# Attention and two MLPs on one core: the value product's halves go through DRAM and are added by GpSimd

## The chip, the cores and the metric

The kernel runs on one core of a Trainium2 chip. The metric is the device time of one execution in microseconds; smaller is better. The kernel before takes 773.73 us (median of 3 runs, 772.16 to 774.55).

## The reference

Three stages follow each other: causal attention over 4 batches x 8 heads with 576 positions and 64 columns a head, an MLP with a softmax gate and a layer norm (512 to 1024 to 512), and an MLP that takes the larger of three products (512 to 768 to 512).

```python
scores = scale * q @ k.T                      # 32 heads, S = 576, D = 64
bias = -(cum[:, :, :, None] - cum[:, :, None, :])
scores = where(causal, -1e9, scores + minimum(bias, 0.0))
attn = softmax(scores);  x = attn @ v         # then to (2304 tokens, 512)
h = x @ w_in                                  # (2304, 1024)
solu = h * softmax(h)
x = (solu - mean) / sqrt(var + 1e-6) * g_ln @ w_out
out = maximum(maximum(x @ w1, x @ w2), x @ w3) @ w_out2
```

## The kernel before

All products run with float32 data that are split in a high part, which is exact in the matmul's format, and a low part; one product takes two or three matmuls. The order of each engine is written out by hand, with semaphores between the engines.

The attention runs in slots, one per head. In slot t TensorE computes the scores of head t (and the first part of those of head t+1, `scores_4`), transposes the probabilities of head t-1 in four groups (`turn` 0 to 3, banks 3 and 4 of PSUM) and multiplies those of head t-2 with the values (`values`, lines 436 to 442). The values lie in `v_hl` with their high part in columns 0 to 63 and their low part in 64 to 127, so that the product has the high half in partitions 0 to 63 and the low half in 64 to 127 of a bank. Columns 0 to 319 of a head go to bank 6 (`PV_A`), 320 to 575 to bank 7 (`PV_B`).

The two halves are joined so: ACT copies the low half of each bank to SBUF (`copy_vlo_a`, `copy_vlo_b`, lines 800 to 812, at the end of its slot), and VectorE adds it to the high half in PSUM and writes the sum into `xT` (`add_a`, `add_b`, lines 1030 to 1042, one slot later, between its row maxima and its `pt_low`). `xT` holds x transposed: head 2j+r of a batch lies in partitions 64r to 64r+63 of block j. TensorE waits for these adds before it writes the banks again (lines 482 and 491).

Per slot VectorE further does `q_low`, five row maxima (`row_max`) and four `pt_low`; ACT does four `pt_high`, the split of v, and five exps; GpSimd does `qk_high` and `k_low` of head t+1 and `split_v` of head t-1 (lines 695 to 702). In the last 8 pairs of slots of its loop it also splits a piece of w_in (`split_win`).

SP issues all transfers, in one queue, in the order of its program. `reload(t, par)` (lines 314 to 325) waits until GpSimd and VectorE are done with head t-2, issues the load of q and k of head t in two copies of 288 KB (one for each half of the partitions), waits for `v_lo_ready` (GpSimd's `split_v` of head t-3), issues the two v loads of head t-1, waits for the scores of head t-2 and issues the small aux load. After each pair of reloads a block of the first MLP's weights is loaded (512 KB of w_in four times, 256 KB of w_out eight times). At the end (lines 359 to 377) the reloads of heads 28 to 31 are written out, with the row sums stored to DRAM and loaded back broadcast (`store_rinv`, `load_rinv`) between them. In slot 28 (RTURN) TensorE turns the row sums and VectorE inverts them.

The first MLP works on 6 groups of 384 tokens. GpSimd multiplies a group with the inverse row sums (`divide`, lines 718 to 723; the first one ahead of the last v split of the attention), ACT and VectorE split it (`x_high`, `x_low`), TensorE multiplies (`hidden`), and GpSimd normalizes (`normalize`) before TensorE transposes again. ACT's first `x_high` stands ahead of its slot 32.

Of the kernel before, what the change touches and what calls it, by code (L numbers as in the profile page):

```python
# [5 lines left out]
F32 = mybir.dt.float32  # L6
# [30 lines left out]
def attention_and_mlp(nc, qkT, v, s, w_in, w_out, g_ln, w1, w2, w3, w_out2, out):  # L37
# [25 lines left out]
    QA = 3 * P - PAD  # L63
    QB = S - QA

    PV_A = [(0, J0 + PAD, J0 + 3 * P, 0), (1, J1, J1 + 2 * P, PAD), (2, J2, J2 + P, PAD + P)]
    PV_B = [(0, J0 + 3 * P, J0 + 5 * P, 0), (1, J1 + 2 * P, J1 + 4 * P, 0), (2, J2 + P, J2 + 3 * P, 0),
            (3, J3, J3 + 2 * P, 0), (4, J4, J4 + P, P)]
# [12 lines left out]
    aux_dram = nc.dram_tensor("aux_dram", (HEADS, 8, S), F32, kind="Internal").ap()  # L81
    rsum_dram = nc.dram_tensor("rsum_dram", (HEADS, S), F32, kind="Internal").ap()

    with ExitStack() as ctx:
# [29 lines left out]
        xg = sb(ab_, "xg", [P, KC, GT])  # L114
        win_lo = sb(ab_, "win_lo", [P, KC, FF], F32R)


        with ExitStack() as a:
# [6 lines left out]
            vlo_a = sb(a, "vlo_a", [D, QA])  # L125
            vlo_b = sb(a, "vlo_b", [D, QB])

# [80 lines left out]
        vloa_copied = sem("vloa_copied")  # L208
        vlob_copied = sem("vlob_copied")
        xa_done = sem("xa_done")  # L210
        xb_done = sem("xb_done")
# [72 lines left out]
        def _(sp):  # L284
# [29 lines left out]
            def reload(t, par, known=None):  # L314
# [10 lines left out]
                load_aux(t, par)  # L325

            reload(2, 0, 2)
            reload(3, 1)

            def reload_pair(pair):  # L330
                reload(2 * pair, 0)
                reload(2 * pair + 1, 1)


            with sp.Fori(2, 2 + KC) as pair:
                reload_pair(pair)
                sp.dma_start(stage[:, bass.ds(pair * FF - 2 * FF, FF)], w_in[bass.ds(pair * P - 2 * P, P), :]).then_inc(w_loaded, 16)
# [69 lines left out]
        def _(pe):  # L407
# [51 lines left out]
            def slot(t, par, known):  # L459
# [17 lines left out]
                if live(known, 2):  # L477
                    pe.wait_ge(v_hi_ready, t - 1)
                    pe.wait_ge(v_lo_ready, t - 1)
                    pe.wait_ge(pt_lo_done, 4 * (t - 1))  # L480
                    if known != 2:
                        pe.wait_ge(xa_done, t - 2)
                    values(t, par, 6, PV_A)
# [5 lines left out]
                if live(known, 2):  # L489
                    if known != 2:  # L490
                        pe.wait_ge(xb_done, t - 2)
# [82 lines left out]
            pe.wait_ge(xa_done, HEADS)  # L574
            pe.wait_ge(xb_done, HEADS)
# [70 lines left out]
        def _(pool):  # L646
# [90 lines left out]
            pool.wait_ge(xa_done, HB)  # L737
            pool.wait_ge(xb_done, HB)
# [4 lines left out]
            pool.wait_ge(xa_done, 2 * HB)  # L743
            pool.wait_ge(xb_done, 2 * HB)
# [8 lines left out]
            pool.wait_ge(xa_done, HEADS)  # L753
            pool.wait_ge(xb_done, HEADS)
# [18 lines left out]
        def _(act):  # L773
# [33 lines left out]
            def copy_vlo_b(t, par, known):  # L807

                if known != 2:
                    act.wait_ge(xb_done, t - 2)  # L810
                act.wait_ge(pv_done, 2 * (t - 2) + 2)
                act.activation(vlo_b[:, :], ps[D:P, 7, 0:QB], ACT.Copy).then_inc(vlob_copied, 1)

            def slot(t, par, known):
# [160 lines left out]
        def _(dve):  # L975
# [49 lines left out]
            def columns(t, par, known):  # L1025

                pair = (t - 4 + par) // 2 if known is not None else (t - 4 + par) >> 1
                return (pair % KC) * TOKENS + (pair // KC) * S

            def add_a(t, par, known):  # L1030

                flat = xT[:, :, :].rearrange("p c t -> p (c t)")
                dve.wait_ge(vloa_copied, t - 2)
                dve.tensor_tensor(flat[D * (1 - par):D * (2 - par), bass.ds(columns(t, par, known), QA)], ps[0:D, 6, 0:QA],  # L1034
                                  vlo_a[:, :], ALU.add).then_inc(xa_done, 1)

            def add_b(t, par, known):

                flat = xT[:, :, :].rearrange("p c t -> p (c t)")
                dve.wait_ge(vlob_copied, t - 2)  # L1040
                dve.tensor_tensor(flat[D * (1 - par):D * (2 - par), bass.ds(columns(t, par, known) + QA, QB)], ps[0:D, 7, 0:QB],
                                  vlo_b[:, :], ALU.add).then_inc(xb_done, 1)

# [10 lines left out]
            def slot(t, par, known):  # L1054
# [6 lines left out]
                if live(known, 3):  # L1061
# [186 lines left out]
```

## Time and profile before

| | |
|---|---|
| median of 3 runs | 773.73 us |
| profiled execution | 776.48 us |
| its span, first to last instruction | 774.2 us |
| mean granted TensorE clock | 0.989 of full speed |
| TensorE / its weight loads busy | 720.6 / 664.9 us (93% / 86%) |
| VectorE busy | 418.0 us (54%) |
| ACT busy | 328.5 us (42%) |
| GpSimd busy | 226.3 us (29%) |
| DMA | 45.26 MB, mean 58 GB/s |

The busy shares are averages over the whole span. In the 40 equal slices of the page VectorE is at 9 tenths from the third to the eleventh slice (attention) and between 1 and 6 tenths after the thirteenth (the MLPs), and GpSimd is at 4 to 9 tenths in the first eleven. TensorE is at 8 to 9 in both stages. The DMA engines are at 4 to 6 tenths in the attention, at 0 to 2 later.

### The profile page before, as it was taken

The page shows a single profiled execution, that of the slowest core. Times are in us where ns is not written, and L with a number is a line of the kernel's source. Part 1 is how long each engine was busy: PE and PEld are TensorE (multiplying, and loading weights), DVE is VectorE, ACT ScalarE, POOL GpSimd, SP SyncE. Part 2 cuts the span into 40 slices and gives each one's busy share as a digit, 9 for nine tenths or more (in the row PEclk, how much of TensorE's full clock was granted, in tenths as well). Part 3 has the DMA queues.
Part 4 walks back from the last instruction along what each step waited for, and adds up shares of the span by engine and source line. Part 5 has one row for each costly group of instructions (what it writes and reads, how often), then busy time and mean ns, then how long its engine had stood idle before and what let it go on. Part 6 is the DMA issues. An engine that isn't in the chain of part 4 may idle for free.

```text
span 774.2 us, 12663 instructions
## 1 busy us (share of the span) xinstructions
PE 720.6 (93%) x4248; PEld 664.9 (86%) x4248; DVE 418.0 (54%) x766; ACT 328.5 (42%) x795; POOL 226.3 (29%) x242
## 2 busy tenths in 40 slices
PE   2798898999889899999999999999999999999997
PEld 1787787888777788889898989999989999899995
DVE  8799999999995684635354463612313213132120
ACT  1688788888874443414232242412112112121111
POOL 6665768989742641304040200000000000000000
PEclk9799999999999999999999999999999999999999
DMA  6555455555341101105200022000010010000101
GB/s 136 118 140 153 130 144 131 141 133 137 95 91 42 42 13 29 42 1 145 60 0 0 0 81 83 1 14 28 1 41 1 1 40 1 30 11 0 41 0 41
DMA packets 46579, 45.26 MB, mean 58 GB/s; under 512 B 22164, under 2 KB 37652, under 8 KB 46516
## 3 DMA queue, kind: packets, MB, share of 16 engines
q1 hardware_dynamic: 46548, 44.86, 21.9%
q8 instruction: 18, 0.29, 0.2%
q14 instruction: 13, 0.11, 0.1%
HBM read 39.43 MB, written 5.38 MB: 58 GB/s over the span
## 4 chain that ended last, share of the span: by engine, by line
PE 65%; DVE 10%; DMA 7%; issue 6%; POOL 5%; SPq 4%; ACT 2%; DVEq 0%; POOLq 0%; ACTq 0%
PE ps L606 10%; PE ps L605 10%; PE ps L604 10%; DMA qk_raw<-in_qk_dram 7%; PE ps L536 4%; PE ps L538 4%; PE ps L537 4%; PE ps L524 3%; PE ps L526 3%; PE ps L525 3%; PE ps L617 3%; PE ps L619 3%; PE ps L618 3%; DVE nmax L1007 2%; POOL qk_b L676 2%
## 5 line engine op out<-in xcount | busy, mean ns | idle before, releaser
L606 PE MATMUL ps<-x_lo,w_hi 128*128 (+1 forms) x432 | 144.4, 334 | 0.0
L604 PE MATMUL ps<-x_hi,w_hi 128*128 128x384 f32 x432 | 144.3, 334 | 0.0
L605 PE MATMUL ps<-x_hi,w_lo 128*128 128x384 f32 x432 | 144.3, 334 | 0.0
L788 ACT ACTIVATE probs<-ps,nmax 128x576 f32<-128x576 f32 (+4 forms) x160 | 82.6, 530 | 17.2 <-DVE nmax L1007 17.2
L798 ACT ACTIVATE pt_hi<-ps 128x512 fp32r<-128x512 f32 (+1 forms) x128 | 69.8, 569 | 34.5 <-PE ps L433 28.3
L433 PE MATMUL ps<-ident,probs 128*128 128x128 f32 x480 | 74.3, 286 | 10.4 <-DVE pt_lo L1014 5.8
L440 PE MATMUL ps<-pt_hi,v_hl 128*128 128x256 f32 (+2 forms) x256 | 67.7, 294 | 16.5 <-DVE xT L1034 13.6
L604 PEld LDWEIGHTS ps<-x_hi,w_hi 128*128 128x128 f32 x432 | 81.1, 188 | 0.2
L605 PEld LDWEIGHTS ps<-x_hi,w_lo 128*128 128x128 f32 x432 | 81.1, 188 | 0.2
L606 PEld LDWEIGHTS ps<-x_lo,w_hi 128*128 128x128 f32 x432 | 81.1, 188 | 0.0
L1014 DVE TENSOR_TENSOR pt_lo<-ps,pt_hi 128x512 fp32r<-128x512 f32 (+1 forms) x128 | 78.0, 649 | 4.8 <-ACT pt_hi L798 3.9
L415 PE MATMUL ps<-k_a,q_a 128*128 128x288 f32 (+2 forms) x192 | 64.3, 342 | 14.5 <-DVE rinvT L1052 14.1
L1007 DVE TENSOR_REDUCE nmax<-ps 128x1 f32<-128x576 f32 (+4 forms) x160 | 72.7, 484 | 4.6 <-PE ps L420 3.2
L933 ACT ACTIVATE m_hi<-stage 128x384 fp32r<-128x384 f32 x36 | 18.9, 525 | 124.9 <-DVE stage L1193 124.9
L440 PEld LDWEIGHTS ps<-pt_hi,v_hl 128*128 128x128 f32 x256 | 49.3, 193 | 21.9 <-issue 14.3
L536 PE MATMUL ps<-lnT_hi,wout_hi 128*128 128x384 f32 x192 | 64.4, 335 | 2.7 <-DVE lnT_lo L1138 2.7
L433 PEld LDWEIGHTS ps<-ident,probs 128*128 128x128 f32 x480 | 53.3, 145 | 15.8 <-issue 6.9
L1195 DVE TENSOR_TENSOR m_lo<-stage,m_hi 128x384 fp32r<-128x384 f32 x36 | 20.1, 558 | 82.2 <-ACT m_hi L933 82.2
L538 PE MATMUL ps<-lnT_lo,wout_hi 128*128 128x384 f32 x192 | 64.2, 335 | 0.0
L537 PE MATMUL ps<-lnT_hi,wout_lo 128*128 128x384 f32 x192 | 64.2, 334 | 0.0
L441 PE MATMUL ps<-pt_lo,v_hl 128*128 128x256 f32 (+2 forms) x256 | 61.0, 286 | 0.0
L524 PE MATMUL ps<-win_hi,x_hi 128*128 128x512 f32 x144 | 57.5, 399 | 2.8 <-DVE ln L1122 2.1
(102 smaller groups left out, 1441.5 us busy)
## 6 DMA issues: line engine op xcount, KB each, us to landing
qk_raw<-in_qk_dram SPq DMA_DIRECT2D x64, 288.0 KB, 4.2
rinvB<-rsum_dram SPq DMA_DIRECT2D x24, 192.0 KB, 3.8
stage<-in_moe_w_dram SPq DMA_DIRECT2D x18, 256.0 KB, 4.4
out_dram<-stage SPq DMA_DIRECT2D x18, 256.0 KB, 2.0
v_raw<-in_v_dram SPq DMA_DIRECT2D x32, 128.0 KB, 2.4
stage<-in_moe_w_out_dram SPq DMA_DIRECT2D x14, 256.0 KB, 2.7
stage<-in_moe_w_in_dram SPq DMA_DIRECT2D x4, 512.0 KB, 3.6
aux_dram<-setup SPq DMA_DIRECT2D x1, 576.0 KB, 4.5
```

The lines of the kernel that those rows point to most:

```text
L433: mm = pe.transpose(ps[:, GBANK[g], P * n:P * (n + 1)], probs[1 - par][:, o:o + P], ident[:, :])
L440: pe.matmul(dst, v_hl[par][:, j, :], pt_hi[par][:, a0:a1], start=(n == 0), stop=False)
L524: pe.matmul(dst, x_hi[ab][:, c, :], win_hi[:, c, cols], start=(c == 0), stop=False)
L536: pe.matmul(dst, wout_hi[:, f, cols], lnT_hi[:, f, :], start=(f == 0), stop=False)
L537: pe.matmul(dst, wout_lo[:, f, cols], lnT_hi[:, f, :], start=False, stop=False)
L538: mm = pe.matmul(dst, wout_hi[:, f, cols], lnT_lo[:, f, :], start=False, stop=(f == FB - 1))
L604: pe.matmul(dst, w_hi[f][:, i, c, :], x2_hi[par][:, c, :], start=(c == 0), stop=False)
L605: pe.matmul(dst, w_lo[f][:, i, c, :], x2_hi[par][:, c, :], start=False, stop=False)
L606: mm = pe.matmul(dst, w_hi[f][:, i, c, :], x2_lo[:, c, bass.ds(g * GT, GT)], start=False, stop=(c == KC - 1))
L788: act.activation(dst, SCORES[c], ACT.Exp, bias=nmax[par][:, c:c + 1], accum_out=sums_all[:, c, bass.ds(t, 1)]).then_inc(exp_done, 1)
L1007: dve.tensor_reduce(nmax[par][:, c:c + 1], SCORES[c], AX_XY if c == NCH - 1 else AX_X, ALU.max, negate=True).then_inc(max_done, 1)
L1014: dve.tensor_tensor(pt_lo[1 - par][:, o:o + n], ps[:, GBANK[g], 0:n], f32(pt_hi[1 - par][:, o:o + n]), ALU.subtract).then_inc(pt_lo_done, 1)
```

## The change

Each product is no longer joined on its way out of PSUM. The banks are divided at column 288 instead of 320. ACT copies all 128 partitions of a bank, both halves together, into a new SBUF tile `halves` (two of them, by parity): the first bank's copy stands ahead of three of the slot's exps, the second's at the end of the slot. Before the first of these ACT waits for the store of the head two before. SP stores each head's tile to a new DRAM tensor `x_dram` (288 KB) in `reload`, behind the aux load, five heads later, and reads it back near the end of the attention: the high halves straight into `xT`, one batch at a time (`load_xa`, two transfers of 576 KB), and the low halves group by group into a new tile `xb` (`load_xb`, four transfers of 192 KB). GpSimd adds `xb` to `xT` before each `divide`. VectorE's two adds per head are gone. TensorE waits for ACT's copies instead of VectorE's adds before it writes a bank again. The scratch for dynamic DMAs is set to 4096.

```diff
+    PV_A = [(0, J0 + PAD, J0 + PAD + HALF, 0), (1, J1, J1 + HALF - PAD, PAD), (2, J2, J2 + HALF - P - PAD, P + PAD)]
...
                 sp.wait_ge(scores_done, 3 * (t - 1))
                 load_aux(t, par)
+                if known is None or known >= 5:
+                    store_x(t - 5, 1 - par)
+
+            def store_x(h, par):
+
+                sp.wait_ge(xa_copied, h + 1)
+                sp.wait_ge(x_copied, h + 1)
+                rows = x_dram[bass.ds(h, 1)].rearrange("a p s -> (a p) s")
+                sp.dma_start(rows, halves[par][:, :, :].rearrange("p a b -> p (a b)")).then_inc(x_stored[par], 16)
+
+            def load_xa(b):
+
+                for par in range(2):
+                    sp.wait_ge(x_stored[par], 16 * (b + 1) * HB // 2)
+                for par in range(2):
+                    src = x_dram[HB * b:HB * (b + 1), 0:D, :].rearrange("(j r) d s -> r d j s", r=2)[par]
+                    sp.dma_start(xT[D * par:D * (par + 1), :, S * b:S * (b + 1)], src).then_inc(xa_loaded, 16)
+
+            def load_xb(g):
+
+                if g > 0:
+                    sp.wait_ge(x_added, g)
+                for part in range(2):
+                    b_, s0 = divmod(g * GT + part * GT // 2, S)
+                    for par in range(2):
+                        src = x_dram[HB * b_:HB * (b_ + 1), D:P, s0:s0 + GT // 2].rearrange("(j r) d t -> r d j t", r=2)[par]
+                        dst = xb[D * par:D * (par + 1), :, part * GT // 2:(part + 1) * GT // 2]
+                        sp.dma_start(dst, src).then_inc(xb_loaded, 16)
...
             reload(HEADS - 4, 0)
+            load_xa(0)
             reload(HEADS - 3, 1)
+            load_xb(0)
             reload(HEADS - 2, 0)
+            load_xa(1)
             sp.wait_ge(rinv_done, 1)
             store_rinv(slice(0, LAST))
             reload(HEADS - 1, 1)
@@
             load_rinv(0)
             sp.wait_ge(v_lo_ready, HEADS - 2)
             load_v(HEADS - 1, 1)
+            store_x(HEADS - 5, 1)
+            load_xa(2)
+            store_x(HEADS - 4, 0)
+            store_x(HEADS - 3, 1)
             sp.wait_ge(xg_ready, 1)
             load_rinv(1)
+            load_xb(1)
+            store_x(HEADS - 2, 0)
+            store_x(HEADS - 1, 1)
+            load_xa(3)
...
             for g in range(2, NG):
                 sp.wait_ge(xg_ready, g)
                 load_rinv(g)
+                load_xb(g)
...
             def divide(g, known):
 
+                cols = xT[:, :, bass.ds(g * GT, GT)]
+                pool.wait_ge(xb_loaded, 64 * (g + 1))
+                pool.tensor_tensor(cols, cols, xb[:, :, :], ALU.add).then_inc(x_added, 1)
                 pool.wait_ge(rinvB_loaded, 64 * (g + 1))
                 if known != 0:
                     pool.wait_ge(x_lo_ready, 3 * g)
-                pool.tensor_tensor(xg[:, :, :], xT[:, :, bass.ds(g * GT, GT)], rinvB[:, :, :], ALU.mult).then_inc(xg_ready, 1)
+                pool.wait_ge(x_added, g + 1)
+                pool.tensor_tensor(xg[:, :, :], cols, rinvB[:, :, :], ALU.mult).then_inc(xg_ready, 1)
...
-            def copy_vlo_a(t, par, known):
-
-                if known != 2:
-                    act.wait_ge(xa_done, t - 2)
+            def copy_half_a(t, par, known):
+
+                if known is None or known >= 4:
+                    act.wait_ge(x_stored[par], (t - 2 - par) * 8)
                 act.wait_ge(pv_done, 2 * (t - 2) + 1)
-                act.activation(vlo_a[:, :], ps[D:P, 6, 0:QA], ACT.Copy).then_inc(vloa_copied, 1)
+                act.activation(halves[par][:, 0, :], ps[:, 6, 0:HALF], ACT.Copy).then_inc(xa_copied, 1)
...
                 if live(known, 1):
                     pt_high(2, t, par, known)
                     pt_high(3, t, par, known)
+                if live(known, 2):
+                    copy_half_a(t, par, known)
                 if live(known, 0):
                     exp(t, par, known, 0)
                     exp(t, par, known, 2)
                     exp(t, par, known, 1)
                 if live(known, 2):
-                    copy_vlo_a(t, par, known)
-                    copy_vlo_b(t, par, known)
+                    copy_half_b(t, par, known)
...
-                if live(known, 3):
-                    add_a(t, par, known)
...
-                if live(known, 3):
-                    add_b(t, par, known)
```

Before the first normalization GpSimd now waits for all four `load_xa`, where it waited for the last adds.

## Rows read from the trace of the kernel before

**Rows 1.** The page, part 1: busy us, share of the span, instructions
```profile
PE 720.6 (93%) x4248; PEld 664.9 (86%) x4248; DVE 418.0 (54%) x766; ACT 328.5 (42%) x795; POOL 226.3 (29%) x242
```

**Rows 2.** Windows, 140 to 180 us: busy us by engine, clock, DMA share
```profile
140.00:180.00 40.00, 37.36 (x286) 33.75 (x285) 39.09 (x75) 35.43 (x105) 35.58 (x38) 1.00 0.53 138
```

**Rows 3.** Waits, 100 to 200 us, of all engines and of SP: total, times, longest
```profile
POOL q_a L670 <- DMA qk_raw<-in_qk_dram: 10.3, 7, 2.8
...
PE ps L440 <- DVE xT L1034: 4.4, 10, 0.9
...
SPq L296 <- POOL v_hl L680: 41.7, 15, 4.5
```

**Rows 4.** Chain that ended last, 139 to 153 us: start, us, what
```profile
139.20 4.28 DMA qk_raw<-in_qk_dram
...
143.74 0.08 POOL q_a L670
...
147.52 0.87 POOL v_hl L680
...
148.55 0.47 SPq L296
...
149.90 0.27 SPq L301
...
150.50 0.36 SPq L340
...
151.56 0.50 SPq L292
...
152.26 4.21 DMA qk_raw<-in_qk_dram
```

**Rows 5.** Timeline of SP's queue, 78 to 100 us: start, us
```profile
81.67 0.47 SPq L296 DMA_DIRECT2D v_raw<-in_v_dram  x1
...
95.94 0.47 SPq L296 DMA_DIRECT2D v_raw<-in_v_dram  x1
```

**Rows 6.** Chain that ended last, 78 to 123 us
```profile
85.58 5.29 DMA qk_raw<-in_qk_dram
```

**Rows 7.** The page, part 6: DMA issues, KB each, median us to landing
```profile
out_dram<-stage SPq DMA_DIRECT2D x18, 256.0 KB, 2.0
...
stage<-in_moe_w_out_dram SPq DMA_DIRECT2D x14, 256.0 KB, 2.7
stage<-in_moe_w_in_dram SPq DMA_DIRECT2D x4, 512.0 KB, 3.6
```

**Rows 8.** Groups by form: count, busy us, mean ns, idle before
```profile
L723 POOL TENSOR_TENSOR xg<-xT,rinvB 128x1536 f32<-128x1536 f32 x6 | 21.0, 3507 | 82.5 <-DVE x_lo L1091 82.5
...
L805 ACT ACTIVATE vlo_a<-ps 64x320 f32<-64x320 f32 x32 | 13.9, 434 | 6.8 <-PE ps L441 6.1
...
L812 ACT ACTIVATE vlo_b<-ps 64x256 f32<-64x256 f32 x32 | 11.8, 369 | 1.2 <-PE ps L441 1.2
L1034 DVE TENSOR_TENSOR xT<-ps,vlo_a 64x320 f32 x24 | 11.6, 484 | 0.7
...
L1182 DVE TENSOR_TENSOR x_lo<-xT,x_hi 128x1536 fp32r<-128x1536 f32 x6 | 10.5, 1758 | 4.1 <-ACT x_hi L920 4.1
...
L1041 DVE TENSOR_TENSOR xT<-ps,vlo_b 64x256 f32 x24 | 9.9, 413 | 0.4
```

**Rows 9.** Timeline of ACT, 139 to 153 us: start, us, [idle before, releaser]
```profile
149.83 0.98 ACT L798 ACTIVATE pt_hi<-ps 128x512 fp32r<-128x512 f32 x2 [0.59 <-PE ps L433]
```

**Rows 10.** Timelines of SP, GpSimd and ACT at the end of the attention
```profile
196.42 1.11 SPq L292 DMA_DIRECT2D qk_raw<-in_qk_dram x2
...
202.88 0.67 POOL L670 TENSOR_SCALAR q_a<-qk_raw 128x576 fp32r<-128x576 f32 x1
...
231.41 3.49 POOL L723 TENSOR_TENSOR xg<-xT,rinvB 128x1536 f32<-128x1536 f32 x1
...
235.69 0.62 ACT L857 ACTIVATE x_hi<-xg 128x512 fp32r<-128x512 f32 x1
```

More of the change, by code:

```diff
@@ L81, in attention_and_mlp @@
     aux_dram = nc.dram_tensor("aux_dram", (HEADS, 8, S), F32, kind="Internal").ap()
+    x_dram = nc.dram_tensor("x_dram", (HEADS, P, S), F32, kind="Internal").ap()
     rsum_dram = nc.dram_tensor("rsum_dram", (HEADS, S), F32, kind="Internal").ap()
@@ L114, in attention_and_mlp @@
         xg = sb(ab_, "xg", [P, KC, GT])
+        xb = sb(ab_, "xb", [P, KC, GT])
         win_lo = sb(ab_, "win_lo", [P, KC, FF], F32R)
@@ L124, in attention_and_mlp @@
             nmax = [sb(a, f"nmax{i}", [P, NCH]) for i in range(2)]
-            vlo_a = sb(a, "vlo_a", [D, QA])
-            vlo_b = sb(a, "vlo_b", [D, QB])
+            halves = [sb(a, f"halves{i}", [P, 2, HALF]) for i in range(2)]
             q_a = [sb(a, f"q_a{i}", [P, SP], F32R) for i in range(2)]
@@ L207, in attention_and_mlp @@
         pv_done = sem("pv_done")
[L208 to L211, printed above, removed]
+        xa_copied = sem("xa_copied")
+        x_copied = sem("x_copied")
+        x_stored = [sem(f"x_stored{i}") for i in range(2)]
+        xa_loaded = sem("xa_loaded")
+        xb_loaded = sem("xb_loaded")
+        x_added = sem("x_added")
         sums_turned = sem("sums_turned")
@@ L325, in reload, with reload_pair, load_win @@
                 load_aux(t, par)
-            reload(2, 0, 2)
[L328 to L335, printed above, removed]
+                if known is None or known >= 5:
[20 more added lines that the diff above has]
+                        sp.dma_start(dst, src).then_inc(xb_loaded, 16)
+            reload(2, 0, 2)
+            reload(3, 1, 3)
+            def reload_pair(pair, known=None):
+                reload(2 * pair, 0, known)
+                reload(2 * pair + 1, 1, known and known + 1)
+            def load_win(pair):
+                sp.dma_start(stage[:, bass.ds(pair * FF - 2 * FF, FF)], w_in[bass.ds(pair * P - 2 * P, P), :]).then_inc(w_loaded, 16)
+            reload_pair(2, 4)
+            load_win(2)
+            with sp.Fori(3, 2 + KC) as pair:
                 reload_pair(pair)
-                sp.dma_start(stage[:, bass.ds(pair * FF - 2 * FF, FF)], w_in[bass.ds(pair * P - 2 * P, P), :]).then_inc(w_loaded, 16)
+                load_win(pair)
             with sp.Fori(2 + KC, 2 + KC + FB) as pair:
@@ L490, in slot @@
                     if known != 2:
[L491 removed]
+                        pe.wait_ge(x_copied, t - 2)
                     values(t, par, 7, PV_B)
@@ L798, in pt_high, with copy_half_b @@
                 act.activation(pt_hi[1 - par][:, o:o + n], ps[:, GBANK[g], 0:n], ACT.Copy).then_inc(pt_hi_done, 1)
-            def copy_vlo_a(t, par, known):
-                if known != 2:
-                    act.wait_ge(xa_done, t - 2)
+            def copy_half_a(t, par, known):
+                if known is None or known >= 4:
+                    act.wait_ge(x_stored[par], (t - 2 - par) * 8)
                 act.wait_ge(pv_done, 2 * (t - 2) + 1)
-                act.activation(vlo_a[:, :], ps[D:P, 6, 0:QA], ACT.Copy).then_inc(vloa_copied, 1)
-            def copy_vlo_b(t, par, known):
-                if known != 2:
-                    act.wait_ge(xb_done, t - 2)
+                act.activation(halves[par][:, 0, :], ps[:, 6, 0:HALF], ACT.Copy).then_inc(xa_copied, 1)
+            def copy_half_b(t, par, known):
                 act.wait_ge(pv_done, 2 * (t - 2) + 2)
-                act.activation(vlo_b[:, :], ps[D:P, 7, 0:QB], ACT.Copy).then_inc(vlob_copied, 1)
+                act.activation(halves[par][:, 1, :], ps[:, 7, 0:HALF], ACT.Copy).then_inc(x_copied, 1)
             def slot(t, par, known):
@@ L1023, in invert_sums @@
                 dve.reciprocal(flat, flat).then_inc(rinv_done, 1)
[L1025 to L1042, printed above, removed]
             q_low(0, 0)
```

23 lines of the change are left out of this document (8 added, 15 removed).

## The prediction

> **What bounds the kernel now.** I read the shares of the engines first [rows 1]: TensorE is busy for 93% of the span and VectorE for 54%. Those are averages of two stages. The change works in the first, the attention, which ends near 240 us; behind it TensorE is at work nearly without a gap. So I read one stretch of the attention by itself [rows 2]: of 40 us, VectorE is busy for 39.09, TensorE for 37.36, ACT for 35.43, GpSimd for 35.58. One head takes 6.5 us there (a pair of heads takes 13.06, below), so that VectorE has 6.37 us of work in a slot, TensorE 6.09, ACT 5.76. From this view VectorE is the bound, and a change that takes work from it must pay. The view can't show a chain that goes round through several engines, each of them with a little idle time, so I went on to the waits [rows 3]: GpSimd waits 10.3 us in 7 pieces for the load of q and k, SP's queue waits 15 times, 41.7 us, for GpSimd's `v_hl`, and TensorE 4.4 us for VectorE's add into xT. GpSimd waits for a DMA and SP waits for GpSimd: that is a closed circle if nothing in it has slack.
>
> The chain of waits says whether it has [rows 4]. From 139.20 to 152.26 us it runs: the second half of a q and k load lands after 4.28; GpSimd starts on it at 143.74, works without a gap and ends with the v split at 148.39 (147.52 + 0.87); SP, which waited for that (line 320), issues two v loads from 148.55, the aux row at 149.90, the weight block at 150.50 and the two copies of the next q and k at 151.56 and 152.26. Then the same again. That is one turn in 13.06 us, for two heads, and nothing in it waits for anything outside. Two such circles are interleaved, one per parity; the other one doesn't issue the weight block, but GpSimd splits w_in in it. In the stretch with the 512 KB blocks of w_in the turn is 95.94 - 81.67 = 14.27 us [rows 5] and its load lands after 5.29 instead of 4.2 to 4.3 [rows 6]. So the attention is held by SP, its queue and GpSimd, with VectorE 0.15 us per slot behind (6.53 against 6.37).
>
> **The change part by part.**
> *Removed from VectorE:* the adds `add_a` and `add_b`, 0.484 + 0.413 = 0.90 us a head, 24 + 8 of each [rows 8]. VectorE falls to 5.5 us a slot, and TensorE no longer waits for line 1034 before its value products. In the slots that the circle holds this is worth nothing. It is worth something where SP has no part in the bound: about 4 slots ahead of the first store and about 5 at the end (heads 27 to 31 and the drain). There the next bound is TensorE's 6.09, so 0.4 us a slot (between 0 and 0.9): 9 x 0.4 = -3.6 us.
> *ACT:* two copies of 64x320 and 64x256 (434 and 369 ns) become two of 128x288, about 0.40 each by their size [rows 8]: the same 0.80. The first moves ahead of three exps. ACT idles 0.59 us a slot there for TensorE's turns [rows 9], and the copy fits into it. The last exp still has to be done before TensorE's first turn of the next slot; if the cover is gone, it costs 0.4 us in each such slot. The new wait for `x_stored` (the store of two heads ago) stands ahead of those exps, and so of TensorE's next slot. The store of a head leaves SP at about 150.5 in the terms of rows 4; 256 KB to DRAM land in 2.0 us [rows 7]; ACT ends the two `pt_hi` copies, behind which the new copy stands, at 150.81 [rows 9], and those of the next slot, where the store is wanted, 6.5 later at 157.3. Taken at nothing.
> *TensorE:* the same columns in other pieces (704 + 1152 before, 608 + 1248 now), nothing.
> *SP, the term that decides:* each head's store of 288 KB stands between the aux load and the next q and k load, that is, inside the circle. What is queued behind it is the load for which GpSimd, then VectorE, then TensorE wait. Its price has two sides. The issue: two v issues take 149.90 - 148.55 = 1.35, so 0.67 each, and two more waits some 0.1: 0.75 at least. The transfer: blocks of 512 KB land in 3.6 and of 256 KB in 2.7 us [rows 7], so 256 KB are worth 0.9 and 288 KB 1.0 us; at the rate of the q and k copies (576 KB between 151.56 and 156.47, of which about 2 are fixed as for the 256 KB store) it would be 1.5. Issue and transfer run beside each other, so the delay is the larger and not the sum: 0.75 to 1.5. I take 1.1, nearest to the slope of the weight blocks, with a little for the issue. A gain is excluded: nothing on SP is removed. Stores are issued from head 5's reload to that of 28, 24 of them, one in each turn of either circle: 12 turns x 1.1 = +13.2 us (9 to 18).
> The Trainium skill (DMA: Bandwidth & Descriptors, Anatomy of one DMA — SWDGE (gpsimd) path) gives 2.0 us fixed and the bytes over 436 GB/s, fitted for transfers that GpSimd issues. By that the store's bytes would be 0.68 us, an estimate of the page's, below the issue time, and the term would be 12 x 0.75 = 9. Rows 7 show 0.9 us for 256 KB, a slower rate, and I go by them.
> *The reads back:* SP issues `load_xa(0)` (1152 KB) ahead of head 29's q and k, `load_xb(0)` (768 KB) ahead of head 30's and `load_xa(1)` ahead of head 31's. At 0.9 us per 256 KB the first takes 4.1, at the rate of q and k 5.8; I take 4.7. Head 29's load is issued from 196.42, its second copy at about 197.0, and lands 4.3 later, at 201.3; GpSimd takes it at 202.88 [rows 10], so 1.6 are covered and 3.1 are left. The other two fall beside the slot in which the row sums are turned and inverted, which gives time; I put 0.4 on them (0 to 5). Together +3.5 (0 to 9).
> *GpSimd's add:* it has the size and the kind of the multiplication behind it, 3.5 us [rows 8]. The first one stands between the v split and the multiplication, which now starts at 231.41 and ends at 234.9; ACT takes xg at 235.69 [rows 10], with the rest of its attention work queued behind this. So 3.5 less 0.8 = +2.7 us, and I put 0.2 on the v split of the last head that comes behind: +2.9 (1 to 5). The other five adds run while GpSimd waits; in the MLPs it has work for a small part of the time. Nothing. The last `load_xa` is needed before the first normalization; it lands some 10 us after the last copy, about when GpSimd has finished its weights anyway. Nothing, but a few us if transfers are slow.
> The Trainium skill (GPSIMD Engine Reference, When to use GPSIMD) speaks against this part: elementwise work with two inputs is about half as fast there as on VectorE. The rows agree, 3507 ns against 1758 for the same 128x1536. On VectorE the first add would cost 1.8 less; the forecast doesn't use this.
>
> **Sum:** 13.2 + 3.5 + 2.9 - 3.6 = +16.0 us. The profiled execution took 776.48, so 792.5 by its own time; the median of the runs is 773.73, so 789.7.
>
> **The rivals.**
> 1. *VectorE was the bound after all* (faster). The circle would have slack that the chain hides, for instance because SP's issues can be taken earlier. Then each of some 24 slots goes from 6.53 towards TensorE's 6.09; the copy ahead of the exps takes half of that back, so 24 x 0.22 = -5.3 and -3.6 outside, with +3.5 and +2.9 at the end: 771. With the reads covered it is 768. It decides if the store's issue and bytes land in idle time of SP. For it: 97.7% of VectorE's time. Against it: rows 4 close without a gap, and rows 3 have seven such waits in 100 us. 0.07 for faster; 0.05 that it ends within 0.3%.
> 2. *Transfers are slower than the weight blocks' slope*: stores to DRAM between 256-byte v pieces and rows of 4.6 KB at 1.5 us or more each, and reads at the upper bounds. 12 x 1.6 + 9 + 5 - 3.6 = +30: 803. 0.18.
> 3. *ACT waits for the store* (`x_stored`). If a store takes over 6 us to land, ACT stands ahead of the exps and TensorE behind it. 1 us in each of 24 slots on top of the forecast would be +40: 813. 0.04.
> 4. *The adds go but nothing else moves*, because the circle takes the store in while it waits for v: only the end's 6.4 less 3.6, 776.5. It is the part of 0.04 that stands between rival 1 and the forecast; it counts as slower by 0.36% or same, half each.
> The forecast has 0.62: 781 to 799.
>
> **Chances and range.** Faster by over 0.3% (about what a measurement of this kernel can tell from no change) 0.07, within it 0.07, slower by more 0.86. The range is 775 to 808: it takes in the bounds 9 and 18 of the stores, rival 4 and most of rival 2, and leaves out rival 1, rival 3 and the tail of rival 2, about 0.2 in all.
>
> **What would show it.** Right: a pair of heads takes 14.0 to 14.6 us in the stretch of rows 2 instead of 13.06; VectorE's share falls from 98% to under 85% and TensorE's to about 86%; the wait of GpSimd for q and k grows; the chain still runs DMA, GpSimd, SP with a store in it. At the end GpSimd takes head 29 several us late and ACT waits about 3 us for xg. Wrong: pairs under 13 us, TensorE above 95% in the attention, or a chain that runs through PE and ACT there; ACT waiting for a store; TensorE waiting in the MLPs for xg.

## The result and the profile after

The changed kernel takes 795.36 us (median of 4 runs, 791.04 to 800.43) against 773.69 us: a ratio of 1.0285, 95% interval 1.0221 to 1.0349. It is slower by 21.7 us; forecast were +16.0, slower with a chance of 0.86, and a range of 775 to 808. The profiled execution took 796.19 us, 19.7 more than that of before.

The page, part 1:

```profile
span 794.3 us, 12664 instructions
...
PE 730.3 (92%) x4248; PEld 672.2 (85%) x4248; DVE 395.7 (50%) x702; ACT 328.9 (41%) x795; POOL 251.8 (32%) x248
```

VectorE gave back 22.3 us and 64 instructions [rows 1], and the kernel got slower. (The adds were 28.7 us; the 32 `q_a` of VectorE and its eight `wout_lo` take some 3 us more each than before.) Now the same 40 us as in [rows 2]:

```profile
140.00:180.00 40.00, 35.95 (x267) 31.55 (x264) 33.32 (x60) 34.00 (x100) 33.22 (x35) 1.00 0.62 169
```

TensorE fell from 37.36 to 35.95 us of 40 (90%, where 86% was forecast) and ACT from 35.43 to 34.00: both get less done in the same time. VectorE fell from 39.09 to 33.32, for the most part by its adds. The waits from 100 to 200 us say for what:

```profile
POOL q_a L716 <- DMA qk_raw<-in_qk_dram: 19.4, 8, 3.9
DVE q_a L1046 <- POOL q_a L716: 14.2, 13, 1.8
...
PE ps L480 <- DVE pt_lo L1060: 9.1, 14, 1.4
```

GpSimd waits 19.4 us for q and k instead of 10.3 [rows 3], and what it delays arrives at VectorE and TensorE. TensorE's wait for the adds is gone. No wait of ACT for a store is among them, nor anywhere else in the attention, so the third rival is out. The chain of waits, one turn of the circle of [rows 4]:

```profile
148.81 0.87 POOL v_hl L726
...
149.83 0.47 SPq L297
...
150.49 0.44 SPq L298
...
151.19 0.27 SPq L302
...
151.78 0.36 SPq L335
...
152.46 0.35 SPq L375
...
153.41 0.51 SPq L293
154.03 4.46 DMA qk_raw<-in_qk_dram
...
158.75 0.68 POOL q_a L716
```

It is the old circle with line 335, the store, in it: from 151.78 to the next issue at 152.46 it takes 0.68 us.

A clock for the attention is the start of GpSimd's `q_a`, once per head (line 670 before, 716 after). Two slots are one turn. Over four turns from head 18 to head 26 it takes (182.99 - 130.66) / 4 = 13.08 us before and (186.53 - 131.15) / 4 = 13.85 after. The whole difference of the two spans, +20.1 us, divides at such marks so (rounded):

| from, to | before | after | difference |
|---|---|---|---|
| start to `q_a` of head 6 | 48.79 | 44.70 | -4.1 |
| `q_a` of head 6 to head 28 (11 turns) | 146.89 | 155.03 | +8.1 |
| head 28 to head 31 | 25.41 | 30.03 | +4.6 |
| head 31 to the first normalization (VectorE's reduction) | 31.12 | 35.91 | +4.8 |
| to the first `wout_lo` of VectorE | 17.21 | 17.14 | -0.1 |
| to the first reduction of the second group | 9.81 | 13.62 | +3.8 |
| to the end | 495.0 | 497.9 | +2.9 |

The first row is mostly spread, not the change: in five other profiles of the changed kernel (a1, a2, both of a3 and a7 below, of which only a1 and a7 touch a store ahead of that mark) head 6 starts at 46.08 to 50.35. The end of the attention, on GpSimd and, in the last line, on ACT:

```profile
211.70 0.67 POOL L716 TENSOR_SCALAR q_a<-qk_raw 128x576 fp32r<-128x576 f32 x1 [4.83 <-DMA qk_raw<-in_qk_dram]
...
219.46 0.67 POOL L716 TENSOR_SCALAR q_a<-qk_raw 128x576 fp32r<-128x576 f32 x1 [3.12 <-DMA qk_raw<-in_qk_dram]
...
229.76 0.67 POOL L716 TENSOR_SCALAR q_a<-qk_raw 128x576 fp32r<-128x576 f32 x1 [3.17 <-DMA qk_raw<-in_qk_dram]
...
240.89 3.47 POOL L768 TENSOR_TENSOR xT<-xT,xb 128x1536 f32<-128x1536 f32 x1
244.50 3.44 POOL L773 TENSOR_TENSOR xg<-xT,rinvB 128x1536 f32<-128x1536 f32 x1
...
248.05 0.63 ACT L903 ACTIVATE x_hi<-xg 128x512 fp32r<-128x512 f32 x1 [3.40 <-POOL xg L773]
```

GpSimd waits 3 to 5 us for each of the loads of heads 29, 30 and 31, which stand behind the reads back. Before, it waited for the last of them alone, 1.29 us. The page, part 6, has what these reads take to land, KB each and median us:

```profile
qk_raw<-in_qk_dram SPq DMA_DIRECT2D x64, 288.0 KB, 4.4
x_dram<-halves SPq DMA_DIRECT2D x32, 288.0 KB, 2.1
xT<-x_dram SPq DMA_DIRECT2D x8, 576.0 KB, 6.6
xb<-x_dram SPq DMA_DIRECT2D x24, 192.0 KB, 4.8
```

ACT's first `x_hi` waits 3.40 us for GpSimd's product, which comes behind the first add.

### The profile page after: what moved, and what is told of

Same layout as the page of the kernel before. It is cut to its first block, busy times and chain, and to the rows that moved or that the text cites. A ratio compares the mean times of both kernels' runs of the same rounds, so it can differ in the third digit from the quotient of the medians.

```text
span 794.3 us, 12664 instructions
## 1 busy us (share of the span) xinstructions
PE 730.3 (92%) x4248; PEld 672.2 (85%) x4248; DVE 395.7 (50%) x702; ACT 328.9 (41%) x795; POOL 251.8 (32%) x248
## 4 chain that ended last, share of the span: by engine, by line
PE 64%; DMA 10%; POOL 7%; issue 6%; SPq 6%; DVE 5%; ACT 2%; POOLq 0%; DVEq 0%; ACTq 0%
DMA qk_raw<-in_qk_dram 10%; PE ps L652 9%; PE ps L650 9%; PE ps L651 9%; PE ps L583 4%; PE ps L585 4%; PE ps L584 4%; PE ps L571 3%; PE ps L573 3%; PE ps L572 3%; PE ps L663 3%; PE ps L665 3%; PE ps L664 3%; PE ps L596 2%; POOL qk_b L722 1%
## 5 line engine op out<-in xcount | busy, mean ns | idle before, releaser
L480 PE MATMUL ps<-ident,probs 128*128 128x128 f32 x480 | 79.4, 293 | 35.9 <-DVE pt_lo L1060 29.7
L1053 DVE TENSOR_REDUCE nmax<-ps 128x1 f32<-128x576 f32 (+4 forms) x160 | 70.1, 482 | 7.5 <-PE ps L467 6.4
L487 PE MATMUL ps<-pt_hi,v_hl 128*128 128x288 f32 (+4 forms) x256 | 71.2, 302 | 0.0
L488 PE MATMUL ps<-pt_lo,v_hl 128*128 128x288 f32 (+4 forms) x256 | 64.5, 297 | 0.0
L1218 DVE TENSOR_TENSOR m_lo<-stage,m_hi 128x384 fp32r<-128x384 f32 x36 | 20.1, 558 | 82.2 <-ACT m_hi L979 82.2
L1046 DVE SCALAR_TENSOR_TENSOR q_a<-qk_raw,q_a 64x576 fp32r<-64x576 f32 x32 | 39.4, 1231 | 34.6 <-POOL q_a L716 34.1
```

The source lines that it names most:

```text
L480: mm = pe.transpose(ps[:, GBANK[g], P * n:P * (n + 1)], probs[1 - par][:, o:o + P], ident[:, :])
L487: pe.matmul(dst, v_hl[par][:, j, :], pt_hi[par][:, a0:a1], start=(n == 0), stop=False)
```

## The experiments

"Of after" and "of before" say which kernel was edited. Turns are measured as above, over four turns from about 130 us if nothing else is said. A ratio is the recorded one to the kernel before in the same job; it isn't exactly that of the two medians.

**The store outside the circle (a1, of after).** SP issues the store while it would wait for v anyway.

```diff
                 load_qk(t, par)
+                if known is None or known >= 5:
+                    store_x(t - 5, 1 - par)
...
                 load_aux(t, par)
-                if known is None or known >= 5:
-                    store_x(t - 5, 1 - par)
```

> The changed kernel with one edit: SP issues a head's store right behind the q and k load of the same reload, where it stands idle until GpSimd has split v, instead of behind the aux load. Theory (the store's issue and bytes stand in the circle of SP, DMA and GpSimd): the turn of two heads between 140 and 180 us falls from 13.8 to 13.1 us or less, the attention is 8 us shorter and the time is 786 to 789. Rival (more bytes in the DMA queues slow the loads wherever the store is issued): the turn stays at 13.6 to 13.9 and the time within 2 us of the changed kernel's 795.

Measured: 788.54 us (786.19 to 791.67), ratio 1.0169 (1.0095 to 1.0244) to a before of 774.38. The turn is (180.78 - 128.23) / 4 = 13.14. Bytes and count of the stores are the same; only their place changed, and of the 8.1 us that the changed kernel loses between head 6 and head 28, 6.8 are gone. The stores now take 4.1 us to land instead of 2.1 (medians, page, part 6), where they stand behind the q and k load, and nothing in the attention waits for that. Window 140 to 180:

```profile
140.00:180.00 40.00, 37.71 (x282) 33.35 (x281) 35.18 (x63) 35.16 (x104) 34.76 (x36) 1.00 0.70 183
```

The DMA share is higher than after's (0.70 against 0.62) and yet TensorE does more, so the load on the DMA engines was not what cost.

**Two issues for the same bytes (a7, of after).** The two counts that wait for a store are doubled with it.

```diff
-                sp.dma_start(rows, halves[par][:, :, :].rearrange("p a b -> p (a b)")).then_inc(x_stored[par], 16)
+                flat = halves[par][:, :, :].rearrange("p a b -> p (a b)")
+                for i in range(2):
+                    sp.dma_start(rows[D * i:D * (i + 1), :], flat[D * i:D * (i + 1), :]).then_inc(x_stored[par], 16)
```

> The changed kernel with each head's store issued as two DMAs of 64 partitions, at the same place: the same bytes, one issue more in each turn. Theory (what the store costs is SP's time for the issue, 0.65 us, and the bytes are hidden): the turn of two heads between 130 and 187 us grows from 13.85 to 14.4 or 14.5. Rival (the bytes are what delays the q and k load): it stays within 0.2 us of 13.85.

Measured: 808.73 us in one run, before 775.48. The turn is (189.33 - 129.75) / 4 = 14.90, so the second issue, with no byte more, costs 1.05 a turn. That is more than the 0.55 to 0.65 expected and more than the first issue did (0.77). On SP the pair stands as

```profile
151.53 1.25 SPq L337 DMA_DIRECT2D x_dram<-halves  x2
153.04 1.16 SPq L293 DMA_DIRECT2D qk_raw<-in_qk_dram  x2
```

It is 1.51 us to the issue of q and k, where one store takes 0.63 to the same issue (0.68 where the weight block follows). The loads of q and k take 4.4 us to land as in the changed kernel (medians). With a1 this says that the term is SP's time per issue, not the transfer. 0.2 us of the 1.05 are not explained by it, and it is one run.

**Without VectorE's adds, nothing else (b1, of before).** ACT copies the high half of each bank straight into `xT`; the low half is left out. No DRAM, no GpSimd add.

```diff
-                act.activation(vlo_a[:, :], ps[D:P, 6, 0:QA], ACT.Copy).then_inc(vloa_copied, 1)
+                act.activation(place(t, par, known, 0, QA), ps[0:D, 6, 0:QA], ACT.Copy).then_inc(xa_done, 1)
...
-                if live(known, 3):
-                    add_a(t, par, known)
...
-                if live(known, 3):
-                    add_b(t, par, known)
```

> The kernel before without VectorE's two adds a head: ACT copies the high half straight into xT with two copies of the same width, and the low half of the value product is left out. Nothing goes through DRAM. Theory (circle): the turn of two heads between 140 and 180 us stays at 13.0, VectorE's busy share there falls from 98% to 84%, and the time falls by the relief outside the circle alone, 2 to 5 us, to 769 to 772. Rival (VectorE is the bound): the turn falls to 12.2 to 12.5, towards TensorE's 6.1 us a head, and the time to 760 to 765.

Measured: 771.12 us (10 runs), ratio 0.9943 (0.991 to 0.9977), so -4.4 us by the ratio and -3.3 by the medians (before 774.38). The turn is (178.73 - 126.51) / 4 = 13.06, as before:

```profile
140.00:180.00 40.00, 37.08 (x284) 33.38 (x283) 35.05 (x62) 35.66 (x107) 35.39 (x38) 1.00 0.54 135
```

VectorE is busy 4 us less in 40, and nobody is sooner. This is the plainest evidence against reading 97.7% as a bound. (Its share is 88%, not the 84% expected: a `q_a` of VectorE takes 1175 ns there instead of 990, mean from 130 to 183 us.) What the kernel gains lies at the end of the attention, where the circle doesn't hold: 3.2 us from head 28 to head 31 and 1.1 from there to the first normalization.

**The circle shortened, nothing else (b2, of before).** The weight block is issued behind the q and k load, in SP's wait for v.

```diff
                 load_qk(t, par)
+                if block is not None:
+                    block()
...
-                reload_pair(pair)
-                sp.dma_start(stage[:, bass.ds(pair * FF - 2 * FF, FF)], w_in[bass.ds(pair * P - 2 * P, P), :]).then_inc(w_loaded, 16)
+                reload_pair(pair, lambda: sp.dma_start(stage[:, bass.ds(pair * FF - 2 * FF, FF)],
+                                                       w_in[bass.ds(pair * P - 2 * P, P), :]).then_inc(w_loaded, 16))
```

> The kernel before with the weight blocks of w_in and w_out issued right behind the q and k load of the second head of a pair, where SP stands idle, instead of between the aux load and the next q and k load. Theory (SP's issues there stand in the circle, and VectorE is only 0.15 us a head behind it): the turn of two heads between 130 and 196 us falls from 13.0 to 12.7 or 12.8, VectorE's share rises to 99 to 100%, the turns with w_in fall by 1 us, and the time is 766 to 770. Rival (the circle is closed elsewhere, such as by GpSimd's own work): the turn stays at 13.0 and the time within 1.5 us of 774.

Measured: 773.76 us (10 runs), ratio 0.9975 (0.9955 to 0.9995). The turn is (186.04 - 132.91) / 4 = 13.28, not shorter, and VectorE's share is 96%, not 99. The expectation fell there. It held for the turns with w_in: the three from head 6 to head 12 take 13.17 us on average instead of 14.11. GpSimd's wait for q and k did shrink, from 10.3 to 4.0 us between 100 and 200, and the chain left the circle. The chain of waits of b2:

```profile
154.15 1.34 DVE q_a L1001
155.52 0.48 DVE nmax L1008
...
156.97 0.49 DVE xT L1035
...
157.60 0.39 PE ps L441
...
158.55 0.79 PE ps L434 x7
```

VectorE's add releases TensorE's value product. So there seems to be a second circle, through VectorE and TensorE with the adds in it, that is about as long as SP's; the next run tests this. VectorE's busy time (6.37 a slot, taken from its share) put it at 12.7; with the idle time inside it, it is 13.1 to 13.3 by b2's turn, and two profiles with the same attention differ by 0.13 (13.08 before, 13.21 in b3 below).

**Both (b4, of before: b1 and b2 together, low half left out).**

> The kernel before with both edits of b1_no_adds and b2_block_in_wait: VectorE without its adds (the low half of the value product is left out) and the weight blocks behind the q and k load. Nothing goes through DRAM. Each edit alone left the turn of two heads at 13.1 to 13.3. Theory (two rings of nearly the same length, one through SP, DMA and GpSimd, one through TensorE, ACT and VectorE with the adds, so that only both edits together pay): the turn falls to 12.1 to 12.5 and the time to 758 to 764. Rival (a third limit at about 13, such as the v split or the scores): the turn stays at 12.9 or more and the time at 768 to 771.

Measured: 758.61 us (756.01 to 759.7), ratio 0.9793 (0.9766 to 0.9819), -16.0 us by the ratio and -16.3 by the medians. The turn is (179.00 - 129.82) / 4 = 12.30:

```profile
140.00:180.00 40.00, 38.53 (x294) 34.47 (x292) 36.55 (x66) 36.83 (x110) 37.45 (x40) 1.00 0.57 137
```

By the ratios one edit alone is worth 4.4 us, the other 1.9, both together 16.0. Two circles of nearly equal length hide each other.

**The reads back later (a2, of after).** `load_xa(0)` and `load_xb(0)` behind the last q and k load, `load_xa(1)` behind the last v load.

```diff
             reload(HEADS - 4, 0)
-            load_xa(0)
             reload(HEADS - 3, 1)
-            load_xb(0)
             reload(HEADS - 2, 0)
-            load_xa(1)
...
             reload(HEADS - 1, 1)
+            load_xa(0)
+            load_xb(0)
...
             load_v(HEADS - 1, 1)
+            load_xa(1)
```

> The changed kernel with load_xa(0) and load_xb(0) behind the last reload instead of ahead of the q and k loads of heads 29 and 30, and load_xa(1) behind the last v load. Theory (the big reads delay head 29's load): GpSimd's wait for q and k at slot 28 falls from 4.8 us to nearly nothing and everything behind it comes 4 to 5 us earlier; the profiled span is 789 to 791 against 794.3. Rival (the delay is made good by the slot with the row sums anyway): under 1.5 us.

Measured: 800.12 us in one run, before 774.38: no gain, and the expected time is missed. GpSimd's waits did go as expected: none for head 29 and 0.30 us for head 30. From head 27 to head 31 it takes 227.99 - 199.71 = 28.28 us, against 36.15 after and 31.03 before. So the reads cost 7.9 in these four slots, and what is left under them is 2.8 faster than before, about what b1 gains there (2.4). But then SP has ten issues (2 `xT`, 4 `xb`, 4 `rinvB`) ahead of the last v load, and gives it all back:

```profile
226.17 1.33 SPq L343 DMA_DIRECT2D xT<-x_dram  x2
227.55 2.79 SPq L354 DMA_DIRECT2D xb<-x_dram  x4
230.39 4.68 SPq L392 DMA_DIRECT2D rinvB<-rsum_dram  x4
235.11 0.80 SPq L297 DMA_DIRECT2D v_raw<-in_v_dram  x1
```

The waits from 220 to 262 us show who stood behind: ACT held by a store (the third rival, in one place), then VectorE, TensorE and GpSimd.

```profile
DVE pt_lo L1060 <- ACT pt_hi L845: 14.2, 4, 12.4
POOL v_hl L726 <- ACT v_hl L825: 13.4, 3, 7.2
...
ACT halves L852 <- DMA x_dram<-halves: 9.7, 1, 9.7
```

**GpSimd's third add (a3, of after).** The table has +3.8 us in a place where the forecast had nothing. There GpSimd's add for group 2 falls beside VectorE's eight `wout_lo`. Of the changed kernel, first VectorE, then GpSimd, then TensorE, and last what `--source` says of the eight: shortest, median and longest in ns.

```profile
282.81 9.36 DVE L1128 SCALAR_TENSOR_TENSOR wout_lo<-stage,g_sb,wout_hi 128x512 fp32r<-128x512 f32 x8
...
287.07 3.88 POOL L768 TENSOR_TENSOR xT<-xT,xb 128x1536 f32<-128x1536 f32 x1
...
292.69 2.71 PE L596 MATMUL ps<-ident,ln 128*128 128x128 f32 x12 [3.50 <-DVE lnT_lo L1161]
...
L1128 DVE SCALAR_TENSOR_TENSOR wout_lo<-stage,g_sb,wout_hi x8: 739/742/3928, 282.8 to 291.4; 128x512 fp32r<-128x512 f32 x8
```

Before, the eight took 6.17 and TensorE waited 0.23. Most of the eight are as quick as ever: one of them takes 3.93 us, about as long as the whole add. Before, one took 1.53. A GpSimd `ln` runs beside them in both kernels and takes 2.95 us instead of the 1.20 of the others, so 6.17 is perhaps not quite their time alone. The edit holds this one add until VectorE is through:

```diff
+                if isinstance(g, int) and g == 2:
+                    pool.wait_ge(wout_lo_ready, 1)
                 pool.wait_ge(xb_loaded, 64 * (g + 1))
```

It ran in two jobs, once and four times:

> The changed kernel, but GpSimd's add for group 2 waits until VectorE has finished the low parts of w_out. Theory (the add and VectorE's scalar_tensor_tensor with two SBUF inputs hold each other up; it took 9.4 us instead of 6.2 for 8 of them): L1128's 8 instructions take 6.2 to 6.6 us again, TensorE's idle time ahead of the transposes falls by 3 us and the span by 3 to 4 us, to about 791. Rival (the 3 us come from something else, such as the low clock of TensorE or a DMA): VectorE's 9.4 us stay or the span doesn't move by more than 1 us.

> The kernel of a3_add_waits again, timed in rounds: the changed kernel with the add for group 2 behind VectorE's low part of w_out. By the profiles the collision cost 3.8 us on the spot and 3 us behind it, in which TensorE ran at a lower granted clock after its 3.5 us of idle time. Theory: the median is 5 to 7 us under the changed kernel's 795.4, that is 788 to 791. Rival (the part behind the collision is spread between executions and not the collision's): 3 to 4 us, 791.5 to 792.5.

Measured: 790.33 us in one run; in the second job 790.99 (789.58 to 792.22), ratio 1.02 (1.0169 to 1.0231). The profile of the second job shows

```profile
285.58 6.18 DVE L1130 SCALAR_TENSOR_TENSOR wout_lo<-stage,g_sb,wout_hi 128x512 fp32r<-128x512 f32 x8
...
291.84 3.45 POOL L770 TENSOR_TENSOR xT<-xT,xb 128x1536 f32<-128x1536 f32 x1 [1.95 <-DVE wout_lo L1130]
292.28 1.94 PE L596 MATMUL ps<-ident,ln 128*128 128x128 f32 x12 [0.30 <-DVE lnT_lo L1163]
```

The mechanism is right: both operations and TensorE's wait are back at their old lengths. Of the size, 3.2 us of VectorE's time are shown, and 3.8 from the first `wout_lo` to the second group's first reduction; between the medians of separate jobs stand 4.4 us, with intervals that touch.

**The same operation in the kernel before (b3, of before).** One more `tensor_tensor` of 128x1536 on GpSimd behind the third normalization, nothing else of the change but the scratch size (the tile and its memset at the start are new too).

```diff
             group(0, 0, True)
+            pool.wait_ge(xb_step, 1)
+            pool.tensor_tensor(xb[:, :, :], xb[:, :, :], xb[:, :, :], ALU.add)
             group(1, 1)
```

> The kernel before with one more GpSimd instruction, an add of a 128x1536 tile to itself (it isn't used), behind the third normalization, where the changed kernel has its add for group 2. No DMA, no wait and no data are changed. Theory (GpSimd's add and VectorE's 8 instructions for the low part of w_out hold each other up): these 8 (L1128 of the changed kernel) take 9.2 to 9.6 us instead of 6.17, and what follows comes 3 to 4 us later. Rival (the delay in the changed kernel came from its DMAs or its order): 6.2 us and no delay.

Measured: 782.59 us in one run, before 775.48.

```profile
269.86 8.65 DVE L1110 SCALAR_TENSOR_TENSOR wout_lo<-stage,g_sb,wout_hi 128x512 fp32r<-128x512 f32 x8
...
274.13 3.18 POOL L767 TENSOR_TENSOR xb<-xb 128x1536 f32<-128x1536 f32 x1
...
279.04 2.65 PE L551 MATMUL ps<-ident,ln 128*128 128x128 f32 x12 [2.79 <-DVE lnT_lo L1143]
```

The stretch up to the second group's reduction takes 12.86 us instead of 9.81, and the eight take 8.65, a little less than the 9.2 expected. What follows takes 498.1 instead of 495.0; the next paragraphs say that about half of this is the instruction's. One instruction of 3.2 us on the least loaded engine costs about 4.6.

Part of that, and of the last row of the table, goes with TensorE's clock. In 25 us that begin 3 to 4 us ahead of `wout_lo`, the changed kernel and then a3 of the second job (columns as in [rows 2]; the clock is the third number from the right):

```profile
279.00:304.00 25.00, 20.20 (x96) 17.66 (x95) 20.65 (x32) 9.45 (x19) 10.46 (x5) 0.86 0.14 31
```

```profile
282.00:307.00 25.00, 23.25 (x122) 19.99 (x121) 19.97 (x39) 11.65 (x23) 12.59 (x6) 1.00 0.19 42
```

The granted clock is 0.86 where TensorE stood idle for 3.50 us (0.53 from 295 to 300 us, near the lower of its two levels, 1.2 and 2.4 GHz), and 1.00 where it stood for 0.30. So it goes in all thirteen profiles: with 3.46 to 3.50 us of idle time 0.86 in after, a2 and a7 and 0.93 in a1, with 2.79 us 0.86 in b3, and with 0.23 to 0.34 us 1.00 in the eight others. What it costs behind the collision can be read from the second group's first reduction to its third: 15.7 to 16.4 us in the four profiles at 0.86, 14.3 in a1 and in the eight at 1.00. In the changed kernel that is 1.4 us of the +2.9.

The rest is elsewhere. Near the end stands a stretch of the same work (from ACT's copy of one output to that of the next group of three), of the changed kernel and then of the one before:

```profile
743.90:782.92 39.02, 37.22 (x199) 35.69 (x198) 8.92 (x16) 6.10 (x12) 0.00 (x0) 0.96 0.02 7
```

```profile
725.29:762.68 37.39, 35.59 (x199) 34.55 (x198) 8.93 (x16) 6.10 (x13) 0.00 (x0) 1.00 0.02 7
```

TensorE is idle for 1.80 us of it in both, and yet the clock is 0.96 in one and 1.00 in the other: 1.6 us. Eight of the thirteen profiles have the long form (after, a1, a2, a7, b1, b2, b3, c2), five the short one (before, both of a3, b4, c1). b1, b2 and c2 have it with no add beside `wout_lo`, so it can't be laid to the collision; what decides it is not shown.

**All together (c1 and c2, of after).** c1 puts the store and the weight blocks in SP's wait for v, reads back from head 24 on in parts, puts the first add ahead of the v split that waits for ACT, and holds the third add. The first read of the low halves of group 1 moves up too. c2 also cuts the reads into pieces of 288 and 192 KB, one behind each q and k load of heads 16 to 27. From the edit of c2:

```diff
                 load_qk(t, par)
+                if known is None or known >= 5:
+                    store_x(t - 5, 1 - par)
+                if block is not None:
+                    block()
...
+            pieces = [lambda p=p, js=js: load_xa(0, (p,), js) for p, js in halves_a]
+            pieces += [lambda part=part, p=p: load_xb(0, (part,), (p,)) for part in range(2) for p in range(2)]
+            pieces += [lambda p=p, js=js: load_xa(1, (p,), js) for p, js in halves_a]
+            for n, pair in enumerate(range(2 * KC, 2 + KC + FB)):
+                reload_pair(pair, 2 * pair, lambda: both(lambda: load_wout(pair), pieces[2 * n + 1]), pieces[2 * n])
...
+            pool.wait_ge(xa_loaded, 64)
+            join(0)
             slot(HEADS - 1, 1, HEADS - 1)
-            pool.wait_ge(xa_loaded, 32)
```

> The changed kernel with all of SP's movable issues out of the circle: stores and weight blocks right behind the q and k load; the reads back in parts of 576 or 384 KB in the same place, from head 24 on; GpSimd's first add ahead of the split of head 30's v, the add for group 2 behind VectorE's low part of w_out. Theory: the turn of two heads falls to 12.1 to 12.6 us, with TensorE at 97% or more as the next bound, the end costs little, and the time is 762 to 769, below both kernels. Rival (the additional 19 MB slow every load by then): turns of 12.9 or more and a time of 774 or more.

> The combination of c1_all with the reads back in smaller parts and earlier: one part of 288 or 192 KB behind each q and k load from head 16 to 27, none later ahead of a q and k load. Theory (what is left of the reads' price in c1_all is the queue ahead of v's load and the next q and k load): the turn of 15.8 us at 159 to 175 us in c1_all is gone (all turns 12.2 to 13.2), and the time is 763 to 766 against 766.8. Rival (the price goes with the bytes, wherever they are): several turns grow to 13.5 or more and the time stays at 766 to 769.

Measured: c1 766.77 us (764.64 to 768.22), ratio 0.9896 (0.9855 to 0.9936); c2 763.71 us (761.09 to 766.58), ratio 0.9866 (0.9834 to 0.9898). c2 is 1.3% faster than the kernel before and, across two jobs, 4% faster than the changed one. c1's turns are (159.06 - 109.35) / 4 = 12.43 and once 174.87 - 159.06 = 15.81, at its first large read; c2's have no such step (the longest is 13.35), (181.91 - 131.97) / 4 = 12.49. Window 140 to 180 of c2:

```profile
140.00:180.00 40.00, 38.99 (x295) 34.95 (x295) 35.99 (x64) 35.94 (x106) 37.34 (x39) 1.00 0.90 228
```

The DMA share is 0.90, and it costs at most 0.2 us a turn against b4's 12.30. What remains to b4, 5.1 us between the medians, goes with the low half: reads at the end and adds on GpSimd, and a wait of ACT for a store of 2.6 us. It wasn't divided further.

## Why the prediction was right, and where it was not

*What bounds the kernel.* Right for this change: the circle of DMA, GpSimd and SP held the attention (a1, a7, and b1, whose turn doesn't move without the adds). Incomplete: "VectorE 0.15 us per slot behind" took VectorE's busy time for its circle's length. b2 showed that circle at 13.28 a turn, no shorter than SP's, and b4 that both had to go for the turn to fall to 12.30. The forecast didn't suffer, since the change opened VectorE's circle and lengthened the other.

*The stores, +13.2 (9 to 18).* The mechanism was right, the size too large: +0.74 a turn over 11 turns, +8.1, just under the lower bound. The step that failed in it is "the delay is the larger" with the transfer as the larger. The transfer was hidden, since q and k landed in 4.46 instead of 4.21 us, and what is left is 0.68 us of SP's queue. The lower side, the issue, was the value to take. The forecast turn of 14.0 to 14.6 was 13.85. The count was off too: the reloads issue 27 stores, up to that of head 31, and not 24; the last three fall into the slots of the reads. The Trainium skill (DMA: Bandwidth & Descriptors, Anatomy of one DMA — SWDGE (gpsimd) path), by which the bytes are worth less than the issue, would have led to 9, nearer to the measured term than the slope of [rows 7]. Its fit would have 288 KB land in 2.7 us, an estimate by the page, which is for transfers that GpSimd issues; here, issued by SP, they took 2.1.

*The reads back, +3.5 (0 to 9).* They cost 7.9 (a2's four slots against after's). The wait of head 29 was seen, 4.83 against 3.1. The "0.4" for the other two was wrong: heads 30 and 31 waited 3.12 and 3.17. The turning of the row sums was to give them time, but the loads of q and k stood in the same queue behind 768 and 1152 KB, and are the next thing wanted there too.

*VectorE's relief, -3.6.* b1 measured -3.3 to -4.4 for it alone, with no gain where the circle holds. a2 shows 2.8 of it in the last four slots, from under the reads. The part ahead of the first store is not shown: the -4.1 of the table is within the spread of the start, and the profile of after has the earliest start of the six of its kind.

*GpSimd's first add, +2.9 (1 to 5).* ACT waits 3.40 for xg. The stretch grew by 4.8; 1.9 of it have no experiment of their own. In c2, where this add and the reads stand earlier, the stretch takes 31.52 us, 0.4 more than before.

*"The other five adds run while GpSimd waits. Nothing."* This is the step that failed outright: +3.8 on the spot and, with the clock, 1.4 behind. GpSimd did wait there, so its time was free; VectorE's was not. The Trainium skill (SBUF — State Buffer, Who interferes with whom) says that a VectorE instruction with two inputs in SBUF contends with a GpSimd instruction that reads SBUF. The rows agree: `wout_lo<-stage,g_sb,wout_hi` is one, and eight of them take 9.36 us beside the add and 6.18 without it, close to 6.18 + 3.45 one behind the other; one of the eight, 3.93 us long, bears nearly all of it. Rows 8 show VectorE's add from PSUM and its x_lo from SBUF, but not what runs beside them; the place of each new GpSimd instruction in VectorE's timeline should have been looked up.

*ACT's copies and `x_stored` at nothing.* Right: no such wait in the attention. a2 shows that the wait can bite (9.7 us) once a store stands behind large reads; c1 and c2 have one of 2.7 and 2.6.

*The sum.* The profile has -4.1 + 8.1 + 4.6 + 4.8 - 0.1 + 3.8 + 2.9, which is +20.1 before rounding. The forecast's 5 us too many on the stores were offset by 4 too few on the reads, 5 for the unseen add and 1.6 at the end that no term had: that 795.36 lies near 789.7 is in part luck, and the terms were off by more than the sum.

## What to carry to other kernels

A share of 98% is not a bound until removing work shortens the turn: look for closed circles in the chain of waits, measure each one's length with its inner idle time, and expect nothing from shortening one while another is as long. In an issuing queue, count issues between the wait and the load that closes the circle, and place everything else behind that load, in small pieces. An instruction on an idle engine is free only when nothing that runs beside it is held up by it: look up what stands there in the other engines' timelines.

## What the runs showed that was not expected

- Eight VectorE `scalar_tensor_tensor` of 128x512 from two SBUF tiles take 6.17 us with only GpSimd's `ln` beside them, 9.36 beside a `tensor_tensor` of 128x1536 as well and 8.65 beside one whose two inputs are the same tile. It isn't a slower pace: one of the eight takes 3.93 us and the median stays at 0.74. GpSimd's add goes from 3.45 to 3.88 in the first case.
- The same 288 KB in two issues instead of one cost 1.05 us more a turn, while a DMA share of 0.90 (c2) went with a turn only 0.2 longer than a share of 0.57 (b4): 12.49 and 12.30.
- 576 KB from DRAM back to SBUF took 6.6 us to land and 192 KB 4.8 (medians, several at once), against 2.1 for a store of 288 KB.
- 1.6 us near the end come and go between profiles with the granted clock, 0.96 or 1.00 over the same work and the same 1.80 us of idle time.
